# Strassen's scheme for the gate and expert-up products of a fused attention and mixture-of-experts kernel

## What is computed

```python
attn_out = attention(q, k, v, proj)       # 2 batches, 8 heads, 768 tokens, head size 64; keys masked by hash bucket
x = attn_out.transpose(0, 2, 1, 3).reshape(1536, 512)
a = x @ w1                                # gates: 512 -> 1024
b = x @ w2
h = a * b @ w3                            # 1024 -> 1024
x = h @ w_out                             # 1024 -> 512
p = domain_probs / (domain_probs.sum(-1, keepdims=True) + 1e-09)
for e in range(4):                        # experts: 512 -> 1024 -> 512
    out += p[:, e:e+1] * (relu(x @ w1[e]) @ w2[e])
```

## Time and profile before

| | |
|---|---|
| runs | 1069.37, 1071.73 and 1071.80 us, median 1071.73 |
| profiled execution, first to last instruction (span) | 1068.7 us |
| median of the runs less that span | 3.0 us |
| PE busy | 1044.1 us (98%) |
| PE weight loads | 973.8 us (91%) |
| DVE, ACT, POOL busy | 415.4 (39%), 372.3 (35%), 184.8 us (17%) |
| moved by DMA | 56.04 MB |

### The profile page before, as it was taken

The page is one execution under the profiler, slowest core; times in us unless marked ns, Lnnn a source line. Parts: engine busy times, 40 slices in busy tenths (PEclk is TensorE's granted clock), DMA queues, the critical chain, the costliest instruction groups (busy, mean ns, idle before and its releaser), DMA issues.

```text
span 1068.7 us, 15988 instructions
## 1 busy us (share of the span) xinstructions
PE 1044.1 (98%) x5808; PEld 973.8 (91%) x5808; DVE 415.4 (39%) x684; ACT 372.3 (35%) x685; POOL 184.8 (17%) x191
## 2 busy tenths in 40 slices
PE   7989999999988999999999999999999999999998
PEld 6879999999977999999999988999889998899987
DVE  5348888889885110101222211322123221222211
ACT  3248888888883121212411102211022110311100
POOL 4021434334323111111510003000030000300000
PEclk9999999999999999999999999999999999999999
DMA  6523333333214000000310002200022000200000
GB/s 227 161 75 97 109 91 97 109 89 102 76 30 165 1 1 0 0 0 0 99 59 0 0 0 79 79 0 0 0 79 79 0 0 0 79 0 29 29 29 29
DMA packets 25171, 56.04 MB, mean 52 GB/s; under 512 B 3680, under 2 KB 10048, under 8 KB 25152
## 3 DMA queue, kind: packets, MB, share of 16 engines
q1 hardware_dynamic: 25152, 55.80, 16.5%
HBM read 40.01 MB, written 3.19 MB: 40 GB/s over the span
## 4 chain that ended last, share of the span: by engine, by line
PE 73%; issue 16%; POOL 4%; DVE 2%; ACT 2%; DMA 1%; SPq 0%; POOLq 0%; DVEq 0%; ACTq 0%
PE ps L215 18%; PE ps L216 18%; PE ps L217 18%; PE ps L966 5%; POOL hid_lo L437 3%; PE ps L950 3%; PE ps L952 3%; PE ps L979 3%; PE ps L981 2%; PE ps L928 1%; PE ps L923 1%; POOL wa_lo L348 1%; DVE expo L680 1%; ACT expo L482 1%; DMA w_raw<-in_moe_w 1%
## 5 line engine op out<-in xcount | busy, mean ns | idle before, releaser
L215 PE MATMUL ps<-xT_hi,wa_hi 128*128 x640 | 217.5, 340 | 2.8 <-DVE wa_lo L778 2.0
L217 PE MATMUL ps<-xT_hi,wa_lo 128*128 x640 | 215.8, 337 | 0.0
L216 PE MATMUL ps<-xT_lo,wa_hi 128*128 x640 | 215.7, 337 | 0.0
L632 ACT ACTIVATE hid_hi<-ps 128x384 fp32r<-128x384 f32 x128 | 62.6, 491 | 392.5 <-PE ps L217 392.5
L215 PE MATMUL ps<-wb_hi,hid_hi 128*128 128x512 f32 x384 | 149.5, 389 | 0.0
L216 PE MATMUL ps<-wb_lo,hid_hi 128*128 128x512 f32 x384 | 149.5, 389 | 0.0
L217 PE MATMUL ps<-wb_hi,hid_lo 128*128 128x512 f32 x384 | 149.4, 389 | 0.0
L861 DVE SCALAR_TENSOR_TENSOR hid_lo<-ps,hid_hi 128x384 fp32r<-128x384 f32 x128 | 70.9, 557 | 183.8 <-ACT hid_hi L632 183.5
L215 PEld LDWEIGHTS ps<-xT_hi,wa_hi 128*128 128x128 f32 x640 | 120.1, 188 | 4.3 <-issue 3.8
L867 DVE SCALAR_TENSOR_TENSOR acc<-ps,gate,acc 128x512 f32 x48 | 36.0, 751 | 224.7 <-PE ps L217 224.7
L216 PEld LDWEIGHTS ps<-xT_lo,wa_hi 128*128 128x128 f32 x640 | 120.2, 188 | 0.6
(11 more groups left out here) (92 smaller groups left out, 1548.6 us busy)
## 6 DMA issues: line engine op xcount, KB each, us to landing
stage<-in_moe_w SPq DMA_DIRECT2D x40, 512.0 KB, 3.8
w_raw<-in_moe_w SPq DMA_DIRECT2D x8, 512.0 KB, 3.8
raw_q<-in_q SPq DMA_DIRECT2D x16, 192.0 KB, 2.9
raw_k<-in_k SPq DMA_DIRECT2D x16, 192.0 KB, 2.8
raw_v<-in_v SPq DMA_DIRECT2D x16, 192.0 KB, 2.7
q_main<-q_cross SPq DMA_DIRECT2D x16, 192.0 KB, 2.7
k_main<-k_cross SPq DMA_DIRECT2D x16, 192.0 KB, 3.0
q_main<-onehot SPq DMA_DIRECT2D x16, 192.0 KB, 2.7
```

Source lines behind the costliest of these rows:

```text
L215: nc.tensor.matmul(out_ps, lhs_hi, rhs_hi, start=start, stop=False)
L216: nc.tensor.matmul(out_ps, lhs_hi, rhs_lo, start=False, stop=False)
L217: return nc.tensor.matmul(out_ps, lhs_lo, rhs_hi, start=False, stop=stop)
L632: nc.scalar.activation(hid_hi[:, ft, :], ps_up[ft % 4][:, 0:HALF], ACT.Relu)\
```

## The change

**Seven products for eight.** A step now takes two feature tiles (`i` and `i + 4`) and both token halves (`t0`, `t1`) of one batch. The depth of 512 is cut into two halves of two tiles. With weight blocks B11 to B22 and activation blocks A11 to A22, seven products of two depth tiles (6 matmuls of 384 columns each) give the four output quarters c11, c12, c21 and c22, in Winograd's form of the scheme. A step is 42 matmuls, where the same outputs took 48.

**Sums around it.** The combined weight blocks T1 to T4 are made on POOL (`combine`, four subtractions of 256 columns), after a wait on the load. ACT rounds the seven blocks in two instructions (`next_weights_first`, 1024 columns, and `next_weights_rest`, 768), DVE makes the low parts (`both_weights_low`). The combined activations S1 to S4 are made once for each use. In a step the first three products are copied from PSUM by ACT (`keep`), and the last three products are added on PE to the banks of the first three; before the fifth product PE waits for the copy of its bank. Then DVE adds `u_sum`, c21 and c12, POOL adds `v_sum` and c22. The order of the weight work of step `g + 2` and the output work of step `g` is fixed in each engine's program.

**Two sweeps.** All gates and experts run for batch 0, then for batch 1, so every weight is loaded, combined and split twice. The down weights are loaded by rows of 128 into a ring of four (`v2`). Since that ring lies over `wp`, the two parts of `wp` (2 MB each) are stored to HBM early in attention and loaded again between the sweeps. The activations of batch 0 are combined by POOL in attention's pairs 4 to 6, and those of batch 1 by ACT and DVE under the last down product of batch 0.

The core of the diff (the gates use the same functions `sum_kept`, `keep` and so on):

```diff
+    ORDER = ((A11, BANK_A), (S3, BANK_Y), (S1, BANK_X), (S2, BANK_Z), (A22, BANK_Y), (A12, BANK_A), (S4, BANK_X))
...
+            def load_group(g, dram):
...
+                if g >= SLOTS:
+                    sp.wait_ge(w_lo_done, 2 * (g - SLOTS) + 2)
...
+            sp.wait_ge(wp_lo_done, FK)
+            for n, part in enumerate((wp_hi_f, wp_lo_f)):
+                sp.dma_start(wp_kept[n, :, :], part.bitcast(F32)).then_inc(wp_stored, 16)
...
         @block.gpsimd
...
+            def combine(n, turn, g):
...
+                w = w_raw[n]
+                pool.wait_ge(w_loaded[n], 64 * turn + 64)
...
+                nc.gpsimd.tensor_tensor(w[:, T1, :], w[:, B12, :], w[:, B11, :], ALU.subtract).then_inc(w_combined, 1)
+                nc.gpsimd.tensor_tensor(w[:, T3, :], w[:, B22, :], w[:, B12, :], ALU.subtract).then_inc(w_combined, 1)
+                pool.wait_ge(w_combined, 4 * g + 1)
...
+                nc.gpsimd.tensor_tensor(w[:, T2, :], w[:, B22, :], w[:, T1, :], ALU.subtract).then_inc(w_combined, 1)
+                pool.wait_ge(w_combined, 4 * g + 3)
...
+                nc.gpsimd.tensor_tensor(w[:, T4, :], w[:, B21, :], w[:, T2, :], ALU.subtract).then_inc(w_combined, 1)
...
+            def expert(b, e, last):
+                for i in range(FG):
...
+                    sum_kept(step, i % 2)
+                    pool.wait_ge(hid_lo_done, 4 * unit)
+                    last_quarter(step, c22)
+                    if not (last and i + SLOTS >= FG):
...
+                        combine(i % 2, turn, step + SLOTS)
+                    split_v2(b, e, i)
...
         @block.scalar
...
+            def weights_high(n, g, lo, hi, combined):
...
+                act.wait_ge(w_combined, 4 * g + combined)
+                nc.scalar.copy(w_hi[n][:, lo:hi, :], w_raw[n][:, lo + 1:hi + 1, :]).then_inc(w_hi_done, 1)
...
+            def keep(step, s):
...
+                for n in range(3):
+                    act.wait_ge(prod, N_PROD * step + n + 1)
+                    nc.scalar.copy(kept[s][n][:, :], ps[4 * s + n][:, 0:HALF]).then_inc(kept_done, 1)
+
+            def next_weights_first(step, s):
+                act.wait_ge(prod, N_PROD * step + 4)
+                weights_high(s, step + SLOTS, 0, 4, 3)
...
         @block.vector
...
+            def sum_u(step, s):
...
+                dve.wait_ge(prod, N_PROD * step + 4)
+                dve.wait_ge(kept_done, 3 * step + 1)
...
+                nc.vector.tensor_tensor(u_sum[:, :], ps[4 * s + BANK_Z][:, 0:HALF], kept[s][0][:, :], ALU.add)\
+                    .then_inc(u_done, 1)
...
         @block.tensor
...
+            def products(step, s, parts, waits):
...
+                pe.wait_ge(w_lo_done, 2 * step + 1)
+                for k, (part, bank) in enumerate(ORDER):
+                    second = (part, bank) in ORDER[4:]
...
+                    if second:
+                        pe.wait_ge(kept_done, 3 * step + bank + 1)
...
+                    last.then_inc(prod, 1)
```

More of the change, by code:

```diff
@@ new lines, in build_program @@
+        dp_rec = place("dp_rec", [P, B * TILES], F32, fold_at)
+        assert fold_at[0] <= fold_end
+        tmp_at = [cursor[0]]
+        kept = [[place(f"kept{n}_{s}", [P, HALF], F32, tmp_at) for n in range(3)] for s in range(2)]
+        u_sum = place("u_sum", [P, HALF], F32, tmp_at)
+        v_sum = place("v_sum", [P, HALF], F32, tmp_at)
+        c11, c12, c21, c22 = (place(n, [P, HALF], F32, tmp_at) for n in ("c11", "c12", "c21", "c22"))
+        acc_at = [tmp_at[0]]
+        acc = place("acc", [P, TILES, D], F32, tmp_at)
@@ L337, in _ @@
+            store(B - 1, 0, HT)
+            for t in range(HT, TILES):
+                store(B - 1, t, 1)
+            sp.wait_ge(stored, 16 * (2 * (B - 1) + 1 + HT))
         @block.gpsimd
@@ L449, in _ @@
+            for b in range(B):
+                gates(b)
+                pool.wait_ge(y_mm, 2 * DK * (b + 1))
+                nc.gpsimd.memset(acc[:, :, :], 0.0).then_inc(acc_zeroed, 1)
+                with pool.Fori(0, E - 1) as e:
+                    expert(b, e, False)
+                expert(b, E - 1, b == B - 1)
         @block.scalar
         def _(act):
-            def piece_high(number, j, hi):
-                act.wait_ge(stage_loaded[j], 4 * number + 16)
-                nc.scalar.copy(hi[:, j * PIECE:(j + 1) * PIECE], stage[j][:, :]).then_inc(piece_hi, 1)
@@ new lines, in next_weights_rest, with gates @@
+            def next_weights_rest(step, s):
+                act.wait_ge(prod, N_PROD * step + N_PROD)
+                weights_high(s, step + SLOTS, 4, 7, 4)
+            def gates(b):
+                for i in range(FG):
+                    a, unit = gate_step_of(b, 2 * i), UNITS * b + i
+                    keep(a, 0)
+                    next_weights_first(a, 0)
+                    if b and i == 0:
+                        act.wait_ge(stored, 32 * b)
+                    act.wait_ge(prod, N_PROD * a + 6)
+                    nc.scalar.copy(a11[:, :], ps[BANK_A][:, 0:HALF]).then_inc(a11_done, 1)
+                    next_weights_rest(a, 0)
+                    keep(a + 1, 1)
+                    next_weights_first(a + 1, 1)
+                    for n, (src, ft, cols) in enumerate(((c21, i, t1), (c22, i + FG, t1), (c11, i, t0), (c12, i + FG, t0))):
+                        if src is c22:
+                            act.wait_ge(ab22_done, FG * b + i + 1)
+                        else:
+                            act.wait_ge(ab_done, 3 * (FG * b + i) + n + 1 - (n > 1))
+                        nc.scalar.copy(hid_hi[:, ft, cols], src[:, :]).then_inc(hid_hi_done, 1)
+                    next_weights_rest(a + 1, 1)
@@ L648, in _ @@
+            for b in range(B):
+                gates(b)
+                y_parts(b)
+                with act.Fori(0, E - 1) as e:
+                    expert(b, e, False)
+                expert(b, E - 1, b == B - 1)
         @block.vector
@@ L877, in _ @@
+            for b in range(B):
+                gates(b)
+                y_parts(b)
+                dve.wait_ge(acc_zeroed, b + 1)
+                with dve.Fori(0, E - 1) as e:
+                    expert(b, e, False)
+                expert(b, E - 1, b == B - 1)
         @block.tensor
@@ new lines, in products @@
+            def products(step, s, parts, waits):
+                n = s
+                pe.wait_ge(w_lo_done, 2 * step + 1)
+                for k, (part, bank) in enumerate(ORDER):
+                    second = (part, bank) in ORDER[4:]
+                    if k == 4:
+                        pe.wait_ge(w_lo_done, 2 * step + 2)
+                    if second:
+                        pe.wait_ge(kept_done, 3 * step + bank + 1)
+                    if k in waits:
+                        pe.wait_ge(*waits[k])
+                    for kt in range(K2):
+                        cols = slice(kt * P, (kt + 1) * P)
+                        last = mult3(ps[4 * s + bank][:, 0:HALF], w_hi[n][:, k, cols], w_lo[n][:, k, cols],
+                                     parts[0][:, part, kt, :], parts[1][:, part, kt, :],
+                                     not second and kt == 0, kt == K2 - 1, second)
+                    last.then_inc(prod, 1)
@@ L1128, in bucket_codes @@
+            for b in range(B):
+                gates(b)
+                multiply_y(b)
+                with pe.Fori(0, E) as e:
+                    expert(b, e)
 def bucket_codes(bits):
```

871 lines of the change are left out of this document (546 added, 325 removed).

## The result

The changed kernel takes **1193.32 us** (median of four runs, 1190.56 to 1195.99); the kernel before took 1071.76 beside it. The ratio is **1.1135**, 95% interval 1.1108 to 1.1163: 121.6 us slower, where 1154 had been forecast. The time lies inside the range of 1112 to 1207, 39 us above the forecast. The four runs lie in two pairs, about 1190.6 us at mean granted clocks of 0.954 and 0.957 and about 1196.0 at 0.945 and 0.944, and the profile is of one of the upper pair.

The account below looks back on a forecast made before the run. After attention PE's matmul count times spacing was taken as the bound: 683 us of matmuls plus 135 of stalls made 818 for 740 (+78); with +3 and +1 in attention, 1154 us, range 1112 to 1207.

Parts of the forecast that it names:

- the rival with the slow subtraction: DVE's scaled subtraction with both inputs in SBUF takes 0.4 us more each, three a step; 1187 us, chance 0.25.
- the turn of the ring: Expert step: circle of waits through ACT, POOL and DVE takes 11.9 us for PE's 7.39, 4.5 of stall.
- PE saves 50.7: Up products in gates and experts: 2016 matmuls of 384 columns for 2304, the 288 fewer worth 50.7 us.
- Each engine has room, the ring has not: Expert step: ACT 6.0, DVE 6.1, POOL 6.2 us, each under PE's 7.39, but their waits on each other take 11.9.
- Exclusion of DVE and POOL: Instructions reading two SBUF operands wait for each other on DVE and POOL; rival without it 1121 us, chance 0.15.
- The scaled subtraction from SBUF: DVE's c21, c22 and c12 low parts, 384 columns with both inputs in SBUF: taken as 0.56 us each.
- POOL's short sums: POOL's weight sums of 256 columns, taken as 0.73 us each from longer ones.
- I take +3, bounds 0 and +8: Attention: the 4 MB store of `wp` makes head 3's one-hot stacks 3 to 7 us late; counted as +3 us.
- The reload of `wp` under 59 us of gates cost nothing.: Between the sweeps: loading `wp` again is hidden under 59 us of gates, at no cost.
- Gates, 3 to 4 a pair: Gates: PE stalls 3 to 4 us per step pair, three pairs a batch, 23 us in all.
- Experts, 14.7 each: Experts: stalls of 2.4, 4.5, 4.5 and 3.3 us, together 14.7 each; 118 for eight, 110 after the last one's 8 less.
- The clock, 0.03: Rival: PE's granted clock falls because PE is busy only 62% of a step; time passes 1200 us, chance 0.03.

Follow-up runs that it names:

- Experiment 2: Changed kernel with ACT's order in the experts altered: copies and relus first, next step's weights last, down weights rounded behind the second relu; 1114.36 us, ratio 1.0418.
- experiment 5: Changed kernel with fourteen extra matmuls that nobody reads filling PE's waits before the fifth product; 1194.35 us, ratio 1.1140.
- experiment 1: Changed kernel with the low part of the down weights set to zero by a POOL memset instead of subtracted; 1169.20 us, ratio 1.0932.
- Experiment 7: Changed kernel with the store of `wp` in eight transfers of 512 KB, two behind each of four head pairs; 1181.56 us, ratio 1.1024.
- Experiment 6: Changed kernel with the reload of `wp` issued behind the weight loads for the second sweep's gate steps 3 and 4; 1183.46 us, ratio 1.1043.
- experiment 8: Changed kernel with ACT's next weights later in experts and gates, POOL's differences first in the gates, reload later, store in eight pieces; 1075.40 us, ratio 1.0028.

## Why the prediction was right, and where it was off

That the time lies inside the range is in part luck. The range reached to 1207 because of the rival with the slow subtraction, which did not come true; without its 33 us the same additions reach to 1174, and 1193 lies above that. What the prediction had right is the turn of the ring; what it had wrong lies at its edges and around it.

- **PE saves 50.7.** The counts are as forecast: 672 of each of three up products (2016), 384 of each down product, and `y` at 33.8 a batch.
- **Each engine has room, the ring has not.** Right. A step 12.0 for 11.9 (its own links, added up with the hand-overs that it names, give 11.8), an expert 78.7 for 77. Experiment 2 cut the circle by order alone and gained 79. The stall of 4.5 shows as 2.8 idle and the rest as PE's slower pace; experiment 5 shows that in the experts the pace is cover and not cause.
- **Exclusion of DVE and POOL.** Right, experiment 1.
- **The scaled subtraction from SBUF.** Taken as 0.56; this row has it, 562 ns with both inputs in SBUF, where the earlier trace rows has 557 with one in PSUM:

```profile
L1156 DVE SCALAR_TENSOR_TENSOR hid_lo<-c,hid_hi 128x384 fp32r<-128x384 f32 x96 | 51.5, 562 | 153.2 <-ACT hid_hi L830 133.9 <-ACT hid_hi L837 18.9 <-ACT hid_hi L832 0.4
```

  The rival at 1187 falls. In experiment 2 the same 96 instructions took 557 to 1682 ns, median 956, where POOL's sums and differences run beside them; the shortest show that it is the exclusion and not the form. So does, for this case, the rule of the Trainium skill's Vector Engine (DVE) Microarchitecture Reference, section "Points that are easy to get wrong"; the measurement decides.
- **POOL's short sums.** 0.73 was read off longer ones; rows have 0.72 to 0.74.

The terms that were off add to the difference. The sum of durations gave a span of 1151.3 and the profiled one is 1194.2, 42.9 more (the median stands 39 over the forecast; this execution was 2.7 longer than the median, and had 1.8 around its span where the sum took 3.0):

- *"I take +3, bounds 0 and +8"* for the store. The first gate product came at 335.44 for 325.08, +10.4, where the sum had +4: **6.4 too little**. The wait alone was 7.6, within its bounds, and the half pace after it came on top, which no bound held. Experiment 7 gets 10.4 back by the first gate product.
- *"The reload of `wp` under 59 us of gates cost nothing."* **This step failed.** It looked at whether `wp` came in time for `y`, and not at what was queued behind it. The wait is 11.6; the gates of batch 1 lost 28.0 for the 11.5 forecast, 16.5 too little. Experiment 6 gets back 9.9, and 9.6 of it in these gates. The other 7 us are not the reload: with it moved these gates still lost 18.4.
- *Gates, 3 to 4 a pair.* Those of batch 0 lost 17.4 for 11.5, **5.9 too little**. Of this 3.6 is the slow pace of the profiled execution. In the kernels with the same gates they lost 13.8, 2.3 more than forecast.
- *Experts, 14.7 each.* 67.3 and 59.2 for 60.2 and 52.2: **14.1 too little**, 1.8 an expert. A turn of the ring was forecast short by 0.1 only; the rest lies at an expert's edges. In the timeline of PE the steps of the second expert start at 525.47, 532.87, 544.86 and 557.94, the next expert at 604.16. By those the second step stalls 4.6 where 2.4 was forecast, the third 5.7 for 4.5, the fourth and the down product together 6.2 for 7.8: the second step, which was to find the helpers ahead, already pays the whole turn.
- *The clock, 0.03.* That chance was too small: it fell, to 0.84 to 0.94 in the gates and experts above. But its forecast of over 1200 did not follow, since in the experts the fall cost nothing measurable (experiment 5); it cost in attention, and 3.6 us in the first gates of the profiled execution. That a thing happens and that it costs are two questions, and the rival had put them in one.

## What to carry to other kernels

A unit of work that needs less of the bounding engine is worth what the longest circle through the other engines lets through: add the durations along the circle, in the engines' own orders, and not the busy time of each. If the circle is longer, look for the instruction that prepares a later step and stands ahead of one that this step is waiting for; moving it (and the down weights) took no instruction more here and gave 79 us. For every large transfer ask what small one is issued behind it on the same queue.

## What the runs showed of the hardware

- After a wait of about 3 us in the changed kernel some 11 to 18 matmuls ran 0.32 us apart, at the lower of the two clock levels, and then 0.176 again. In experiment 8, with waits of 1.0 to 1.7 us and one of 3.3, none did from the gates' first product on. In the experts, where the ring sets the pace, this cost nothing measurable; in attention it came on top of the wait.
- A transfer of a later step's weights, issued behind 4 MB on SP's queue, kept its reader waiting 11.8 us, though it did not need those 4 MB; with the reload issued two steps later PE's wait of 11.6 behind it was gone.
- Three PSUM copies on ACT back to back took 1.23 us for 3 x 0.48: in a row each costs 0.41.
